# Last stage of an attention, experts and mixing kernel: theta three tiles ahead in the first batch

## The chip, the cores and the metric

The kernel runs on one core of a Trainium2 chip. The metric is the device time in microseconds (us). TensorE (PE in the profile) multiplies matrices and writes to PSUM, a memory of eight banks of 128 x 512 floats; VectorE (DVE), ScalarE (ACT) and GpSimd (POOL) do the elementwise work; SyncE (SP) issues DMAs. Each engine runs its own list of instructions in the order in which it is written and waits on semaphores for the others.

## The reference

Three parts follow one another: attention with a local band, a mixture of experts, and the stage that the change is in. That one is, for x of 2 x 768 x 512:

```python
def _moe2_ref(x, w_theta, w_tok_r, w_tok_i, w_ch):
    theta = x @ w_theta
    cos_t, sin_t = (np.cos(theta), np.sin(theta))
    zr = x * cos_t
    zi = x * sin_t
    yr = np.einsum('ts,bsd->btd', w_tok_r, zr)
    yi = np.einsum('ts,bsd->btd', w_tok_i, zi)
    y = yr + yi
    u = x + y
    return (u + np.maximum(u @ w_ch, 0.0)).astype(np.float32)
```

## The kernel before

The last stage works on `NT` = 12 tiles of 128 tokens, `QT` = 6 for each of the two batches. Products are made exact enough by splitting every operand into a high and a low part (`exact`, line 1192: three matmuls, high x high and the two mixed ones, for each piece). ScalarE writes the high part, VectorE subtracts it from the whole for the low part.

For one tile n the work goes:

- VectorE `weigh(n)` (line 958): multiplies the gathered rows by the expert's probability, in `x_tok`.
- PE `turn_x2(n)` (L1243): four transposes of the tile into PSUM bank 6.
- ACT `x_high(n)` (L634) and DVE `x_low(n)` (L961): the halves `x2T_hi`, `x2T_lo`, two buffers each.
- PE `theta(n)`: 12 matmuls of 512 columns (`wth_hi`, `wth_lo` with `x2T_hi`, `x2T_lo`) into bank 7.
- DVE `reduce_angle(n)` (L988 to L995, "the angles" below): six dependent instructions that read bank 7 and bring theta into a range for the sine. Its last one counts `s_e_rr`.
- ACT `rotation(n)` (L640, L641, L643): Abs and two Sin; DVE `rotate(n)` (L968): x times cosine and sine; inside it stands `weigh(n + 2)`; ACT `z_high(n)` (L648), DVE z_lo (L961).
- PE `mix(n, 0)` and `mix(n, 1)`: 18 matmuls each, the tile's part of the token mix for all six output tiles of its batch, accumulated in banks 0 to 5.

When a batch's six tiles are mixed, VectorE adds x (`add_y`, L1001), PE turns u (`turn_u`, L1281), its halves are made (`u_high`, `u_low`), and `channels(n)` multiplies by w_ch; `finish` (L1006) writes the output tile. The weights of the token mix are split too, one block of 128 rows of both matrices at a time (`weights_high(m)`, L663 and L664, `weights_low(m)`), w_ch last (m = 6).

The order is written out by hand in each engine's list. PE begins with turn_x2(0), theta(0), turn_x2(1), theta(1), turn_x2(2). Then step s is: mix(s, 0); turn_u(s - 6) from s = 6 on; theta(s + 2); turn_x2(s + 3); mix(s, 1); channels(s - 6). VectorE's step s, which starts from -2, works with m = s + 2: reduce_angle(m), x_low(m + 1), weights_low(m + 1) while m is 2 to 5, rotate(m). For m = 0 and 1 the weight split stands behind rotate. ScalarE's list has the same form. `theta(n)` waits for `s_e_rr` at n, that is for the angles of tile n - 1, since all thetas share bank 7.

Of the kernel before, what the change touches and what calls it, by code (L numbers as in the profile page):

```python
# [25 lines left out]
P = 128  # L26
# [96 lines left out]
def channel_bank(n):  # L123

    return 7 if n < QT else n % QT

# [7 lines left out]
def program(nc, q2, kx, vx, n_global, n_local, w_gates, w_experts, w_theta, w_tok_rT, w_tok_iT, w_ch,  # L134
# [5 lines left out]
    with ExitStack() as ctx:  # L140
# [402 lines left out]
        def _(act):  # L543
# [87 lines left out]
            def x_high(n):  # L631
                act.wait_ge(s_e_tx, n + 1)
                wait(act, s_e_th, n - 1)
                act.copy(x2T_hi[:, n % 2, :, :], ps[:, 6, :].rearrange("p (c q) -> p c q", c=DC)).then_inc(s_e_xh, 1)  # L634
# [34 lines left out]

            act.activation(ang_a[:, 0:1], half_pi[:, 0:1], ACT.Sin)  # L670
            x_high(0)
            weights_high(0)
            for s in range(-2, NT):
                m, n = s + 2, s - QT
                if n >= 0:
                    u_high(n)
                if m + 1 < NT:
                    x_high(m + 1)
                if 2 <= m < QT:
                    weights_high(m + 1)  # L680
                if m < NT:
                    rotation(m)
                    z_high(m)
                if m < 2:
                    weights_high(m + 1)
# [5 lines left out]
        def _(dve):  # L691
# [271 lines left out]
            def rotate(n):  # L963

                dve.wait_ge(s_e_trig, 2 * (n + 1))
                wait(dve, s_e_zl, n)
                for m in range(2):
                    dve.tensor_tensor(z[:, m, :], x_tok[:, n, :], trig[:, m, :], ALU.mult).then_inc(s_e_z, 1)  # L968
                if n + 2 < NT:
                    weigh(n + 2)  # L970
                dve.wait_ge(s_e_z, 2 * (n + 1))
                dve.wait_ge(s_e_zh, n + 1)
                low(z_lo[:, n % 2, :, :], z[:], z_hi[:, n % 2, :, :]).then_inc(s_e_zl, 1)

            def x_low(n):
                dve.wait_ge(s_e_xh, n + 1)
                low(x2T_lo[:, n % 2, :, :], ps[:, 6, :].rearrange("p (c q) -> p c q", c=DC), x2T_hi[:, n % 2, :, :]).then_inc(s_e_xl, 1)
# [6 lines left out]
            def reduce_angle(n):  # L984
                dve.wait_ge(s_e_th, n + 1)
                th = ps[:, 7, :]
# [31 lines left out]
            low(wth_lo[:], wth[:], wth_hi[:]).then_inc(s_w_lo, 1)  # L1018
            weigh(0)
            weigh(1)  # L1020
            x_low(0)
            weights_low(0)
            for s in range(-2, NT):
# [5 lines left out]
                if m + 1 < NT:  # L1029
                    x_low(m + 1)  # L1030
# [3 lines left out]
                if 2 <= m < QT:  # L1034
                    weights_low(m + 1)
                if m < NT:
                    rotate(m)
                if m < 2:
                    weights_low(m + 1)
# [13 lines left out]
        def _(pe):  # L1053
# [184 lines left out]
            def turn_x2(n):  # L1238
                pe.wait_ge(s_x2, n + 1)
                wait(pe, s_e_xl, n)  # L1240
                wait(pe, s_e_ul, n - QT - 2)
                for c in range(DC):
                    last = pe.transpose(ps[:, 6, c * P:(c + 1) * P], x_tok[:, n, c * P:(c + 1) * P], ident)  # L1243
                last.then_inc(s_e_tx, 1)

            def theta(n):
                pe.wait_ge(s_e_xl, n + 1)
                wait(pe, s_e_rr, n)
# [3 lines left out]
                exact(ps[:, 7, :], [((x2T_hi[:, n % 2, c, :], x2T_lo[:, n % 2, c, :]), (wth_hi[:, c, :], wth_lo[:, c, :]))  # L1252
                                    for c in range(DC)], True, True).then_inc(s_e_th, 1)

            def mix(n, part):
# [7 lines left out]
                for i in range(QT):  # L1263
                    if part == 0 and n == QT:
# [8 lines left out]
            def turn_u(n):  # L1273
                pe.wait_ge(s_e_u, n + 1)
                if n < QT:
                    pe.wait_ge(s_e_xl, min(n + QT + 3, NT))
# [19 lines left out]
            for n in range(2):  # L1296
                theta(n)
                turn_x2(n + 1)
            for s in range(NT):
# [3 lines left out]
                if s + 2 < NT:  # L1303
                    theta(s + 2)
                if s + 3 < NT:
                    turn_x2(s + 3)
# [55 lines left out]
```

## Time and profile before

| what | us |
|---|---|
| median of 3 runs | 564.17 |
| lowest, highest | 562.51, 564.87 |
| the profiled execution | 563.1 |
| its span in the trace | 561.2 |
| PE busy in the span | 496.5 |
| DVE busy | 287.0 |
| ACT busy | 197.0 |

The profile is of one execution. Busy time is the time in which an engine executes; matmuls are pipelined and overlap their neighbours, so the start of one to the start of the next tells what it costs. "Idle before" in a row is the time in which the engine did nothing, with the work that ended the wait. The granted clock is the share of 2.4 GHz that TensorE had: 1.00 is 2.4 GHz, 0.50 is 1.2 GHz.

The last stage begins when the rows of the experts have come back, about 365 us into the span, and lasts to the end.

### The profile page before, as it was taken

The numbers are of one execution on the slowest core, as the hardware profiler recorded it, in microseconds if no ns is written. First come the engines' busy times: TensorE is split into PE (matmuls) and PEld (weight loads), VectorE is DVE, ScalarE is ACT, GpSimd is POOL, SyncE is SP. The second block draws the span as 40 slices with busy tenths as digits, with TensorE's granted clock in tenths as the row PEclk, the third lists the DMA queues.
The fourth block names the chain that finished last, engine by engine and source line by source line (L and its number), as shares of the span: only waits on it lengthen the run. The fifth ranks groups of instructions, "written<-read, shape, count | busy, mean of one in ns | idle before, by whom it ended". The sixth has DMA issues, their size and how long they took to land.

```text
span 561.2 us, 9141 instructions
## 1 busy us (share of the span) xinstructions
PE 496.5 (88%) x3228; PEld 420.0 (75%) x3229; DVE 287.0 (51%) x641; ACT 197.0 (35%) x411; POOL 113.3 (20%) x111
## 2 busy tenths in 40 slices
PE   0799999922699999999999999558999999999987
PEld 0577777711699999999899899446888878888866
DVE  5577887546411514141442531257988685655053
ACT  2588877602011313131423411334544322222010
POOL 3977773000111222121222211000000000000000
PEclk9999999965699999999999999877999999999999
DMA  7533344476331547382992800150000000000012
GB/s 268 201 137 107 118 145 161 189 255 273 107 110 39 227 182 277 136 339 76 380 378 76 347 36 19 33 196 0 1 0 2 0 0 20 20 19 20 19 39 94
DMA packets 19842, 70.76 MB, mean 126 GB/s; under 512 B 3038, under 2 KB 3294, under 8 KB 15712
## 3 DMA queue, kind: packets, MB, share of 16 engines
q1 hardware_dynamic: 16880, 64.05, 30.0%
q0 software_dynamic: 2640, 6.30, 3.2%
q8 instruction: 17, 0.28, 0.2%
q14 instruction: 17, 0.14, 0.1%
q10 hardware_dynamic: 288, 0.00, 0.0%
HBM read 62.21 MB, written 10.49 MB: 130 GB/s over the span
## 4 chain that ended last, share of the span: by engine, by line
PE 80%; DVE 8%; DMA 6%; issue 3%; ACT 1%; SPq 0%; POOLq 0%; DVEq 0%; POOL 0%
PE ps L1192 42%; PE ps L1220 18%; PE ps L1066 5%; PE ps L1124 5%; PE ps L1108 4%; DMA w_sb<-in_w_experts 4%; PE ps L1088 3%; PE ps L1206 1%; PE ps L1281 1%; PE ps L1243 1%; DMA xin<-x_rows,rows_in 1%; DVE glob L723 1%; DMA x_tok<-y_rows 0%; PE ps L1199 0%; SPq L437 0%
## 5 line engine op out<-in xcount | busy, mean ns | idle before, releaser
L1220 PEld LDWEIGHTS ps<-xT,w_sb 128*128 128x128 f32 x1024 | 118.2, 194 | 3.8 <-issue 1.4
L1220 PE MATMUL ps<-xT,w_sb 128*128 128x128 f32 x1024 | 118.8, 277 | 1.6 <-DVE xT L950 1.0
L936 DVE SCALAR_TENSOR_TENSOR hT_lo<-ps,hT_hi 128x512 fp32r<-128x512 f32 x32 | 22.1, 691 | 101.1 <-ACT hT_hi L613 101.0
L945 DVE TENSOR_TENSOR w_lo<-w_sb,w_hi 128x1024 fp32r<-128x1024 f32 x32 | 37.0, 1220 | 39.0 <-ACT w_hi L624 39.0
L1192 PE MATMUL ps<-w_hi,hT_hi 128*128 128x512 f32 x128 | 51.5, 402 | 0.0
L567 ACT ACTIVATE prob<-raw,row_min 128x256 f32<-128x256 f32 (+1 forms) x96 | 46.2, 484 | 13.4 <-DVE row_min L786 12.3
L1192 PE MATMUL ps<-w_hi,hT_lo 128*128 128x512 f32 x128 | 50.1, 391 | 0.0
L1192 PE MATMUL ps<-w_lo,hT_hi 128*128 128x512 f32 x128 | 49.9, 390 | 0.0
L613 ACT ACTIVATE hT_hi<-ps 128x512 fp32r<-128x512 f32 x32 | 19.1, 598 | 83.1 <-PE ps L1220 83.1
L617 ACT COPY yout<-ps 128x512 f32<-128x512 f32 x16 | 9.4, 587 | 85.2 <-PE ps L1192 85.2
L786 DVE CUSTOM_DVE_ANT_0 raw<-ps,levels 128x256 f32<-128x256 f32 (+1 forms) x96 | 33.8, 394 | 4.8 <-PE ps L1066 4.8
L624 ACT CAST w_hi<-w_sb 128x1024 fp32r<-128x1024 f32 x32 | 31.1, 1046 | 12.8 <-DVE slot_part L906 12.8
L1066 PE MATMUL ps<-k_hi,q_hi 64*128 64x256 f32 (+1 forms) x96 | 19.1, 394 | 16.9 <-POOL k_lo L492 15.8
L492 POOL TENSOR_TENSOR k_lo<-k_raw,k_hi 128x1344 fp32r<-128x1344 f32 (+1 forms) x16 | 28.9, 1829 | 14.1 <-ACT k_hi L552 14.1
L1124 PE MATMUL ps<-probT,v_sb 128*64 128x128 f32 x352 | 30.5, 291 | 0.2
L1108 PE MATMUL ps<-cst,prob 128*128 128x128 f32 x176 | 30.1, 292 | 0.2 <-ACT prob L567 0.2
L1192 PE MATMUL ps<-z_hi,wti_hi 128*128 128x512 f32 x72 | 29.2, 405 | 0.0
L1192 PE MATMUL ps<-z_hi,wtr_hi 128*128 128x512 f32 x72 | 28.2, 392 | 0.6 <-DVE x_tok L1001 0.6
L1066 PEld LDWEIGHTS ps<-k_hi,q_hi 64*128 64x128 f32 x96 | 9.6, 196 | 24.9 <-issue 20.5
L1192 PE MATMUL ps<-z_hi,wti_lo 128*128 128x512 f32 x72 | 28.2, 392 | 0.0
L1192 PE MATMUL ps<-z_lo,wti_hi 128*128 128x512 f32 x72 | 28.1, 390 | 0.0
L1192 PE MATMUL ps<-z_hi,wtr_lo 128*128 128x512 f32 x72 | 28.0, 389 | 0.0
(185 smaller groups left out, 948.6 us busy)
## 6 DMA issues: line engine op xcount, KB each, us to landing
w_sb<-in_w_experts SPq DMA_DIRECT2D x32, 1024.0 KB
v_sb<-in_vx SPq DMA_DIRECT2D x8, 640.0 KB, 4.0
k_raw<-in_kx SPq DMA_DIRECT2D x8, 432.0 KB, 5.4
q_raw<-in_q SPq DMA_DIRECT2D x8, 384.0 KB, 6.0
x_rows<-x_tok SPq DMA_DIRECT2D x2, 1536.0 KB, 8.9
x_tok<-y_rows SPq DMA_DIRECT2D x12, 256.0 KB, 5.2
out_x<-o_sb SPq DMA_DIRECT2D x12, 256.0 KB, 2.0
wtr<-in_w_tok_rT SPq DMA_DIRECT2D x6, 384.0 KB
```

The source lines that it names most:

```text
L492: last_part = pool.tensor_tensor(low, whole, high.bitcast(F32), ALU.subtract)
L567: act.activation(where, of, ACT.Exp, bias=row_min[:, m:m + 1], scale=-1.0, accum_out=den[:, h % 2, i, b:b + 1]).then_inc(s_exped, 1)
L613: act.activation(hT_hi[:, 4 * half:4 * half + 4, :], ps[:, 1 + half, :].rearrange("p (c q) -> p c q", c=4), ACT.Relu).then_inc(high, 1)
L624: act.copy(w2_hi_quarter(q), quarter(w_sb, par, q)).then_inc(s_w2_hi, 1)
L786: dve.tensor_tensor_reduce(raw[:, g % 2, b * WINDOW:b * WINDOW + w], ps[:, 2 * (g % 2) + b, 0:w], levels[:, h, min(i, 1), 0:w], -DH ** -0. ...
L936: dve.scalar_tensor_tensor(hT_lo[:, part, :], ps[:, 1 + half, :].rearrange("p (c q) -> p c q", c=4), 0.0, hT_hi[:, part, :].bitcast(F32), ...
L945: dve.tensor_tensor(quarter(w_lo, par, q), quarter(w_sb, par, q), w2_hi_quarter(q).bitcast(F32), ALU.subtract).then_inc(s_w2_lo, 1)
L1066: last = pe.matmul(bank, of[d, r, i * P:(i + 1) * P], part, start=(m == 0), stop=(m == 2))
L1108: last = pe.transpose(ps[:, 4 + r, c], prob[:, r, c], ident)
L1124: last = pe.matmul(ps[b * DH:(b + 1) * DH, 6, (i % GROUP) * P:(i % GROUP + 1) * P], v_sb[:, h % 2, b, block, :], probT[:, r, b * WINDOW + ...
L1192: last = pe.matmul(bank, a, b, start=(start and j == 0 and m == 0), stop=(stop and j == count - 1 and m == 2))
L1220: last = pe.matmul(ps[:, 1 + half, f * P:(f + 1) * P], w_sb[:, par, c // 2, j:j + P], xT[:, c, :], start=(c == 0), stop=(c == DC - 1))
```

## The change

The change alters the lists of PE, ACT and DVE in the last stage. Everything ahead of it is the same.

- PE's list begins with turn_x2(0), turn_x2(1), theta(0), turn_x2(2), theta(1), theta(2), turn_x2(3). In steps 0 to 5 it has theta(s + 3) and turn_x2(s + 4), in step 6 neither, and from step 7 on the same as before.
- theta(1) writes bank 5 and turn_x2(1) bank 4. These are banks of the mix, so the first mix waits before bank 5 until the angles of tile 1 are reduced. All other thetas stay in bank 7, all other turns in bank 6.
- theta(1) does not wait for `s_e_rr`, theta(2) waits for 1, and theta(n) from 3 on for n, as before.
- DVE's list: the split of the first weight block comes ahead of the first `weigh`; three tiles are weighed at the start, and `rotate(n)` weighs tile n + 3; x_low of the tile that `x2_at(s)` names (m + 2 in the first batch) comes behind reduce_angle(m), then the weight split, then the rotation. ACT's list follows.

```diff
--- before.py
+++ after.py
@@ -123,6 +123,26 @@
 def channel_bank(n):
 
     return 7 if n < QT else n % QT
+
+
+def theta_bank(n):
+
+    return 5 if n == 1 else 7
+
+
+def x2_bank(n):
+
+    return 4 if n == 1 else 6
+
+
+def theta_at(s):
+
+    return [s + 3] if s < QT else [s + 2] if QT < s < NT - 2 else []
+
+
+def x2_at(s):
+
+    return [s + 4] if s < QT else [s + 3] if QT < s < NT - 3 else []
 
 
 def wait(eng, sem, value):
@@ -631,7 +651,7 @@
             def x_high(n):
                 act.wait_ge(s_e_tx, n + 1)
                 wait(act, s_e_th, n - 1)
-                act.copy(x2T_hi[:, n % 2, :, :], ps[:, 6, :].rearrange("p (c q) -> p c q", c=DC)).then_inc(s_e_xh, 1)
+                act.copy(x2T_hi[:, n % 2, :, :], ps[:, x2_bank(n), :].rearrange("p (c q) -> p c q", c=DC)).then_inc(s_e_xh, 1)
 
             def rotation(n):
 
@@ -667,22 +687,24 @@
                     act.copy(wch_hi[:], wch[:]).then_inc(s_w_hi, 1)
 
 
+            weights_high(0)
             act.activation(ang_a[:, 0:1], half_pi[:, 0:1], ACT.Sin)
             x_high(0)
-            weights_high(0)
+            x_high(1)
+            weights_high(1)
+            x_high(2)
             for s in range(-2, NT):
                 m, n = s + 2, s - QT
                 if n >= 0:
                     u_high(n)
-                if m + 1 < NT:
-                    x_high(m + 1)
-                if 2 <= m < QT:
+                if m:
+                    for ahead in x2_at(s):
+                        x_high(ahead)
+                if 0 < m < QT:
                     weights_high(m + 1)
                 if m < NT:
                     rotation(m)
                     z_high(m)
-                if m < 2:
-                    weights_high(m + 1)
             for n in range(QT, NT):
                 u_high(n)
 
@@ -966,15 +988,15 @@
                 wait(dve, s_e_zl, n)
                 for m in range(2):
                     dve.tensor_tensor(z[:, m, :], x_tok[:, n, :], trig[:, m, :], ALU.mult).then_inc(s_e_z, 1)
-                if n + 2 < NT:
-                    weigh(n + 2)
+                if n + 3 < NT:
+                    weigh(n + 3)
                 dve.wait_ge(s_e_z, 2 * (n + 1))
                 dve.wait_ge(s_e_zh, n + 1)
                 low(z_lo[:, n % 2, :, :], z[:], z_hi[:, n % 2, :, :]).then_inc(s_e_zl, 1)
 
             def x_low(n):
                 dve.wait_ge(s_e_xh, n + 1)
-                low(x2T_lo[:, n % 2, :, :], ps[:, 6, :].rearrange("p (c q) -> p c q", c=DC), x2T_hi[:, n % 2, :, :]).then_inc(s_e_xl, 1)
+                low(x2T_lo[:, n % 2, :, :], ps[:, x2_bank(n), :].rearrange("p (c q) -> p c q", c=DC), x2T_hi[:, n % 2, :, :]).then_inc(s_e_xl, 1)
 
             def u_low(n):
                 dve.wait_ge(s_e_uh, n + 1)
@@ -983,7 +1005,7 @@
 
             def reduce_angle(n):
                 dve.wait_ge(s_e_th, n + 1)
-                th = ps[:, 7, :]
+                th = ps[:, theta_bank(n), :]
                 wait(dve, s_e_trig, 2 * (n - 1))
                 then(dve.tensor_scalar(ang_k[:], th, float(1 / (2 * np.pi)), MAGIC, ALU.mult, ALU.add))
                 then(dve.tensor_scalar(ang_k[:], ang_k[:], MAGIC, None, ALU.subtract))
@@ -1016,27 +1038,28 @@
 
             dve.wait_ge(s_w_hi, 1)
             low(wth_lo[:], wth[:], wth_hi[:]).then_inc(s_w_lo, 1)
+            weights_low(0)
             weigh(0)
             weigh(1)
+            weigh(2)
             x_low(0)
-            weights_low(0)
+            x_low(1)
+            weights_low(1)
             for s in range(-2, NT):
                 m, n = s + 2, s - QT
                 if n >= 0:
                     u_low(n)
                 if m < NT:
                     reduce_angle(m)
-                if m + 1 < NT:
-                    x_low(m + 1)
+                for ahead in x2_at(s):
+                    x_low(ahead)
                 if s == QT - 1:
                     for i in range(QT):
                         add_y(i)
-                if 2 <= m < QT:
+                if 0 < m < QT:
                     weights_low(m + 1)
                 if m < NT:
                     rotate(m)
-                if m < 2:
-                    weights_low(m + 1)
                 if n >= 0:
                     finish(n)
             add_y(QT)
@@ -1237,19 +1260,21 @@
 
             def turn_x2(n):
                 pe.wait_ge(s_x2, n + 1)
-                wait(pe, s_e_xl, n)
-                wait(pe, s_e_ul, n - QT - 2)
+                if n > 1:
+                    pe.wait_ge(s_e_xl, n if n > 2 else 1)
+                wait(pe, s_e_ul, n - QT - 2 if n > QT + 3 else 0)
                 for c in range(DC):
-                    last = pe.transpose(ps[:, 6, c * P:(c + 1) * P], x_tok[:, n, c * P:(c + 1) * P], ident)
+                    last = pe.transpose(ps[:, x2_bank(n), c * P:(c + 1) * P], x_tok[:, n, c * P:(c + 1) * P], ident)
                 last.then_inc(s_e_tx, 1)
 
             def theta(n):
                 pe.wait_ge(s_e_xl, n + 1)
-                wait(pe, s_e_rr, n)
+                if n > 1:
+                    pe.wait_ge(s_e_rr, n if n > 2 else 1)
                 wait(pe, s_e_o, n - QT - 2)
                 if n == 0:
                     pe.wait_ge(s_w_lo, 1)
-                exact(ps[:, 7, :], [((x2T_hi[:, n % 2, c, :], x2T_lo[:, n % 2, c, :]), (wth_hi[:, c, :], wth_lo[:, c, :]))
+                exact(ps[:, theta_bank(n), :], [((x2T_hi[:, n % 2, c, :], x2T_lo[:, n % 2, c, :]), (wth_hi[:, c, :], wth_lo[:, c, :]))
                                     for c in range(DC)], True, True).then_inc(s_e_th, 1)
 
             def mix(n, part):
@@ -1261,6 +1286,8 @@
                     if b == 0:
                         pe.wait_ge(s_w_lo, n + 2)
                 for i in range(QT):
+                    if part == 0 and n == 0 and i == theta_bank(1):
+                        pe.wait_ge(s_e_rr, 2)
                     if part == 0 and n == QT:
                         pe.wait_ge(s_e_u, i + 1)
                     q = slice(i * P, (i + 1) * P)
@@ -1273,7 +1300,7 @@
             def turn_u(n):
                 pe.wait_ge(s_e_u, n + 1)
                 if n < QT:
-                    pe.wait_ge(s_e_xl, min(n + QT + 3, NT))
+                    pe.wait_ge(s_e_xl, min(max(n, 1) + QT + 3, NT))
                 wait(pe, s_e_ul, n if n <= QT else n - 1)
                 if n > QT:
                     pe.wait_ge(s_e_o, QT)
@@ -1293,17 +1320,20 @@
                        for c in range(DC)], True, True).then_inc(s_e_v, 1)
 
             turn_x2(0)
-            for n in range(2):
-                theta(n)
-                turn_x2(n + 1)
+            turn_x2(1)
+            theta(0)
+            turn_x2(2)
+            theta(1)
+            theta(2)
+            turn_x2(3)
             for s in range(NT):
                 mix(s, 0)
                 if s >= QT:
                     turn_u(s - QT)
-                if s + 2 < NT:
-                    theta(s + 2)
-                if s + 3 < NT:
-                    turn_x2(s + 3)
+                for ahead in theta_at(s):
+                    theta(ahead)
+                for ahead in x2_at(s):
+                    turn_x2(ahead)
                 mix(s, 1)
                 if s >= QT:
                     channels(s - QT)
```

The order of TensorE's instructions at the start of the stage, before (`x_tok` is turned, `wth` times `x2T` is theta):

```order
L1243 MATMUL ps<-cst,x_tok 128x128 [waits x2]
L1243 MATMUL ps<-cst,x_tok 128x128 x3
L1192 MATMUL ps<-wth_hi,x2T_hi 128x512 [waits w_lo,e_xl]
L1192 MATMUL ps<-wth_lo,x2T_hi 128x512
L1192 MATMUL ps<-wth_hi,x2T_lo 128x512
```

and in the changed kernel:

```order
L1267 MATMUL ps<-cst,x_tok 128x128 [waits x2]
L1267 MATMUL ps<-cst,x_tok 128x128 x3
L1267 MATMUL ps<-cst,x_tok 128x128 [waits x2]
L1267 MATMUL ps<-cst,x_tok 128x128 x3
L1215 MATMUL ps<-wth_hi,x2T_hi 128x512 [waits w_lo,e_xl]
```

A second turn has come between the first and theta(0).

TensorE at the end of mix(0, 0), before, where theta(2) follows:

```order
L1192 MATMUL ps<-z_hi,wtr_hi 128x512
L1192 MATMUL ps<-z_lo,wtr_hi 128x512
L1192 MATMUL ps<-z_hi,wtr_lo 128x512
L1192 MATMUL ps<-wth_hi,x2T_hi 128x512 [waits e_rr,e_xl]
L1192 MATMUL ps<-wth_lo,x2T_hi 128x512
```

and in the changed kernel, where theta(3) follows:

```order
L1215 MATMUL ps<-z_lo,wtr_hi 128x512
L1215 MATMUL ps<-z_hi,wtr_lo 128x512
L1215 MATMUL ps<-z_hi,wtr_hi 128x512 [waits e_rr]
L1215 MATMUL ps<-z_lo,wtr_hi 128x512
L1215 MATMUL ps<-z_hi,wtr_lo 128x512
L1215 MATMUL ps<-wth_hi,x2T_hi 128x512 [waits e_rr,e_xl]
L1215 MATMUL ps<-wth_lo,x2T_hi 128x512
```

The rows at the end are alike; what moved is the tile. The wait `e_rr` of the last rows is for 2 before and for 3 in the change, and the mix has a wait of its own ahead of its last three matmuls.

VectorE from x_low of the first step (s = -2) on, before (`z` is the rotation's product, `ang` the angles):

```order
L961 TENSOR_TENSOR x2T_lo<-ps,x2T_hi 128x512 [waits e_xh]
L968 TENSOR_TENSOR z<-x_tok,trig 128x512 [waits e_trig]
L968 TENSOR_TENSOR z<-x_tok,trig 128x512
L958 TENSOR_SCALAR x_tok<-x_tok,p_sel 128x512 [waits gathered2]
L961 TENSOR_TENSOR z_lo<-z,z_hi 128x1024 [waits e_zh,e_z]
L961 TENSOR_TENSOR wtr_lo<-wtr,wtr_hi 128x768 [waits w_hi]
L961 TENSOR_TENSOR wti_lo<-wti,wti_hi 128x768
L988 TENSOR_SCALAR ang_k<-ps 128x512 [waits e_th]
```

and in the changed kernel:

```order
L983 TENSOR_TENSOR x2T_lo<-ps,x2T_hi 128x512 [waits e_xh]
L990 TENSOR_TENSOR z<-x_tok,trig 128x512 [waits e_trig]
L990 TENSOR_TENSOR z<-x_tok,trig 128x512
L980 TENSOR_SCALAR x_tok<-x_tok,p_sel 128x512 [waits gathered3]
L983 TENSOR_TENSOR z_lo<-z,z_hi 128x1024 [waits e_zh,e_z]
L1010 TENSOR_SCALAR ang_k<-ps 128x512 [waits e_th]
L1011 TENSOR_SCALAR ang_k<-ang_k 128x512 [waits ch]
L1013 SCALAR_TENSOR_TENSOR ang<-ang_k,ps 128x512 [waits ch]
L1015 SCALAR_TENSOR_TENSOR ang<-ang_k,ang 128x512 [waits ch]
L1016 SCALAR_TENSOR_TENSOR ang<-ang_k,ang 128x512 [waits ch]
L1017 TENSOR_SCALAR ang<-ang 128x512 [waits ch]
L983 TENSOR_TENSOR x2T_lo<-ps,x2T_hi 128x512 [waits e_xh]
```

The weight split (`wtr_lo`, `wti_lo`) of this place has moved ahead; the angles follow z_lo directly. The first `x2T_lo` is of tile 1 before and of tile 2 in the change, and the last row is the one of tile 3.

## Rows read from the trace of the kernel before

**Rows 1.** The page's first line: span and instructions
```profile
span 561.2 us, 9141 instructions
```
**Rows 2.** Waits of TensorE, 366 to 562 us: total, times, longest
```profile
PE ps L1192 <- DVE x2T_lo L961: 7.4, 3, 4.0
```
**Rows 3.** Timeline of PE: start us, us, line, operation, shape, count, [idle before]
```profile
377.16 0.50 PE L1192 MATMUL ps<-wth_hi,x2T_hi 128*128 128x512 f32 x1 [4.04 <-DVE x2T_lo L961]
...
382.10 0.50 PE L1192 MATMUL ps<-z_hi,wtr_hi 128*128 128x512 f32 x1
...
388.39 0.72 PE L1192 MATMUL ps<-wth_hi,x2T_hi 128*128 128x512 f32 x1 [1.95 <-DVE x2T_lo L961]
...
393.20 0.48 PE L1192 MATMUL ps<-z_hi,wti_hi 128*128 128x512 f32 x1
...
401.48 0.39 PE L1192 MATMUL ps<-wth_hi,x2T_hi 128*128 128x512 f32 x1
...
404.20 0.60 PE L1243 MATMUL ps<-cst,x_tok 128*128 128x128 f32 x4
...
450.05 0.48 PE L1192 MATMUL ps<-z_hi,wti_hi 128*128 128x512 f32 x1
...
466.96 0.39 PE L1192 MATMUL ps<-wch_hi,uT_hi 128*128 128x512 f32 x1
```
**Rows 4.** Busy time by stretch of the last stage, PEclk the granted clock
```profile
365.60:368.10 2.50, 1.11 (x4) 0.71 (x4) 1.18 (x2) 1.34 (x3) 0.00 (x0) 0.50 0.98 320
373.10:377.10 4.00, 0.02 (x1) 0.00 (x0) 3.83 (x7) 1.15 (x3) 0.00 (x0) 1.00 0.00 0
377.10:378.30 1.20, 1.14 (x5) 0.97 (x6) 0.00 (x1) 1.20 (x3) 0.00 (x0) 0.98 0.07 14
378.30:381.50 3.20, 3.20 (x9) 2.36 (x8) 2.38 (x4) 1.84 (x3) 0.00 (x0) 0.50 0.00 0
386.40:388.40 2.00, 0.05 (x2) 0.01 (x1) 1.87 (x4) 0.62 (x2) 0.00 (x0) 1.00 0.00 0
388.40:391.50 3.10, 3.10 (x8) 2.42 (x9) 1.69 (x3) 1.74 (x4) 0.00 (x0) 0.52 0.00 0
```
**Rows 5.** Timeline of ACT, same columns as rows 3
```profile
376.54 0.63 ACT L640 ACTIVATE ang_a<-ang 128x512 f32<-128x512 f32 x1 [2.80 <-DVE ang L995]
...
404.83 0.59 ACT L634 CAST x2T_hi<-ps 128x512 fp32r<-128x512 f32 x1 [1.25 <-PE ps L1243]
...
405.32 0.84 ACT L663 CAST wtr_hi<-wtr 128x768 fp32r<-128x768 f32 x1
...
406.06 0.83 ACT L664 CAST wti_hi<-wti 128x768 fp32r<-128x768 f32 x1
...
408.65 0.64 ACT L640 ACTIVATE ang_a<-ang 128x512 f32<-128x512 f32 x1 [1.76 <-DVE ang L995]
...
428.06 1.92 ACT L667 CAST wch_hi<-wch 128x2048 fp32r<-128x2048 f32 x1
```
**Rows 6.** Timeline of DVE, same columns as rows 3
```profile
378.33 1.29 DVE L968 TENSOR_TENSOR z<-x_tok,trig 128x512 f32<-128x512 f32 x2 [1.23 <-ACT trig L643]
...
380.81 1.23 DVE L961 TENSOR_TENSOR z_lo<-z,z_hi 128x1024 fp32r<-128x1024 f32 x1 [0.79 <-ACT z_hi L648]
...
403.69 1.22 DVE L961 TENSOR_TENSOR z_lo<-z,z_hi 128x1024 fp32r<-128x1024 f32 x1 [0.79 <-ACT z_hi L648]
...
404.83 0.68 DVE L988 TENSOR_SCALAR ang_k<-ps 128x512 f32<-128x512 f32 x1
...
409.13 0.95 DVE L961 TENSOR_TENSOR wtr_lo<-wtr,wtr_hi 128x768 fp32r<-128x768 f32 x1
...
410.00 0.95 DVE L961 TENSOR_TENSOR wti_lo<-wti,wti_hi 128x768 fp32r<-128x768 f32 x1
...
431.45 2.28 DVE L961 TENSOR_TENSOR wch_lo<-wch,wch_hi 128x2048 fp32r<-128x2048 f32 x1
...
454.20 3.67 DVE L1001 TENSOR_TENSOR x_tok<-ps,x_tok 128x512 f32<-128x512 f32 x6
```

## The prediction

> **What bounds the kernel now.** I read the page's head first, then the waits of TensorE in the last stage, then the last stage in order of time on TensorE, VectorE and ScalarE, and at last the granted clock of single stretches. One execution spans 561.2 us and its time is 563.1 us, 1.9 outside the span [rows 1]. From 366 us on TensorE lacks work in few places: 7.4 us in three waits for a low half of the turned x (`x2T_lo`) [rows 2]. Two of the three lie where the change works: theta(1) starts at 377.16 after 4.04 idle, theta(2) at 388.39 after 1.95 [rows 3]. From mix(0,1) at 393.20 to mix(5,1) at 450.05, five steps, TensorE is dense: 56.85 / 5 = 11.37 us a step [rows 3]. The clock reads 1.00 in the idle 2.0 us before 388.4 and 0.52 in the 3.1 us behind it; after the 4.0 us idle it is 0.98 for 1.2 us and 0.50 for 3.2; after the 7.4 us idle at the start it is 0.50 as well [rows 4]. So behind each idle stretch about 3.2 us of matmuls ran at 1.2 GHz instead of 2.4, about 1.6 to 1.7 us lost each time.
>
> **The opening.** What is hoisted costs nothing: the first weight split goes before the first gathered tile, where TensorE waits for `x_tok` anyhow. turn_x2(1) goes beside ScalarE's and VectorE's work between turn_x2(0) and theta(0), a gap in which TensorE idles. Theta(1) no longer waits for the first angles, since its bank is 5; theta(2), behind it in bank 7, does: it takes the slot at 377.16 that theta(1) had. That removes one theta from later, and the long idle before it. But mix(0,0) waits for z_lo(0), which hangs on theta(0), angles(0) and the rotation, and none of these moves; z_lo starts at 380.81 [rows 6], mix(0,0) at 382.10 [rows 3] in both kernels. So the gain of the opening isn't banked at mix(0,0); it would be at theta(2)'s old place.
>
> **The loop the change closes.** Bank 7 holds every theta from 2 on. Theta(3), behind mix(0,0) in TensorE's order, must wait for the angles of tile 2 (`s_e_rr` at 3). Before, theta(2) stood there and wanted the angles of tile 1 alone. In general, step s now runs theta(s+3), which wants angles(s+2), and behind it turn_x2(s+4). On VectorE x_low(s+4) stands ahead of the weight split, of rotate(s+2) and so of angles(s+3), for which theta(s+4) waits. Every link waits for the one before, so one step of TensorE can't be shorter than the sum:
> - theta start to x_high start 3.35 (401.48 to 404.83) [rows 3, 5];
> - x_high and two casts of ScalarE 0.49 + 2 x 0.74 = 1.97, then Abs to the rotation's product 1.79 (376.54 to 378.33) [rows 5, 6]: 7.1. VectorE's own leg: the casts end at about 5.4, then two splits 0.87 apart [rows 6], 7.2. The later counts: 7.2;
> - product to z_lo 2.48 (378.33 to 380.81), z_lo to the next angles 1.14 (403.69 to 404.83), angles to their end 3.82 (404.83 to 408.65) [rows 5, 6].
>
> That is 14.6 us against TensorE's 11.37. In the step with w_ch the cast takes 1.92 and the split 2.2 [rows 5, 6], so the product comes at 3.35 + 0.49 + 1.92 + 2.2 = 8.0 and the loop is 15.4; in the step without weights the product comes at 5.6 and the loop is 13.1. Before, theta(s+3) needed angles(s+2) as well, but these ran while TensorE did mixes, and x_low stood only behind a turn that had been issued before; nothing in a step waited for the next theta but its own angles.
>
> **The sum.** Angles(1) start 381.95 (380.81 + 1.14), end 385.77. x_low(3) 0.6 and two splits 1.74 put the product at 388.0; + 2.48 + 1.14 + 3.8 makes angles(2) end and theta(3) start at 395.4. (Mix(0,0) itself waits some 0.3 in its last bank for angles(1), inside the same gap.) TensorE, done with mix(0,0) at about 386.7, idles 8.7 us. From there five loops: 3 x 14.64 + 15.4 + 13.1 = 72.4, so theta(8) starts at 467.8 and mix(5,1) 3.07 later (theta 2.72, turn 0.35) at 470.9, 20.8 us later than before. Given back: theta(8) and turn_x2(9), once in step 6, are done. Before, channels(0) came 16.9 us after mix(5,1) began (450.05 to 466.96) [rows 3]. Before, VectorE was still at angles(7) when the banks were ready and made the six additions in one piece, 3.67 us from 454.20 on [rows 6]. Now it is idle there: the additions follow the banks (the last matmul at 4.15, one addition 0.6 to 0.7) and end at 5.0; product to z_lo and its own time, 2.48 + 1.14, make 8.6; turn_u(0) at 8.3 and its halves (0.6, 0.6, 0.6) 10.1; angles(8) end at 13.9, and channels(0) waits for these: 3.0 back. Behind this both kernels have the same order and TensorE is dense. Net at full clock: +17.8.
>
> The clock on top. Theta(3) follows 8.7 us idle and would run at 1.2 GHz: its 12 matmuls and the turn 2.8 more (as theta(0) after 7.4 idle, whose clock was 0.50) [rows 4]. Theta(4) to theta(7) follow idles of 14.6 - 11.4 = 3.2 and once 4.0; the row after 1.95 and the one after 4.04 both lost 1.7 in the next theta, 4 x 1.7 = 6.8, and since theta is a link of the loop, that lengthens the loop. Theta(8) follows 1.7, I count nothing (else 1.7). Not shown by the trace is a stall of that size in every step; bounds from the nearest rows: 0 below (dense stretches show 1.00) and 1.7 on six thetas above. I take 9.6. The sum is +27.4: 563.1 + 27.4 = 590.5, and since the median of the runs shown is 1.1 above the profiled one, 591.
>
> The Trainium skill (TensorE: Matmul & The Clock Gate, HAM oscillation) has the same thing at work where a matmul stream is interrupted at every repetition: the clock falls back each time. The row after 1.95 us idle agrees [rows 4]; the sum above holds without the page.
>
> **The rivals.**
> 1. The stall is paid once. VectorE needs less than TensorE for a tile (in the steady part it waits for theta), so after theta(3) it might stay ahead. Then mix(0,1) starts at 398.5 or with the slow clock 401.3 instead of 393.20: 5 to 8, less what step 6 returns: about 570. Against it: x_low(s+4) can't start before turn_x2(s+4), and rotation and angles are queued behind it. 5%.
> 2. The loop as computed, but the clock stays at 2.4 GHz behind stalls of 3.2 us: 17.8 + 2.8 = 20.6, so 585; against it is the row after 1.95 idle. 18%.
> 3. The clock spreads into the mixes so that TensorE's own work, not only theta, passes the loop: 14.6 + 1.7 against 8.7 us of other work at half clock, 17.4 + 5.5: up to 6 more in some steps; 600 and over. 6%.
> 4. Faster: the look-ahead holds. If theta(3) needed no bank that VectorE still has to read, it would follow mix(0,0) at 386.7 and mix(0,1) start at 389.8 instead of 393.20: 3.4 less, so 561. It decides on the row of theta(3): idle below 2 us. For it: nothing but that x_low(3) is done by then. The Trainium skill (Perfetto Trace Analysis, Optimizing Tensor Performance) advises to rotate independent matmul groups through different PSUM banks so that the reading of one lies beside the next; by it the own bank of theta(1) is a gain. No trace here shows two thetas side by side, and from theta(2) on one bank is used. 4%.
>
> The forecast has 67%.
>
> **How the numbers follow.** 591 is the forecast's; its own spread is the clock's (0 to 1.7 for each of the last thetas, 588 to 594). The range takes in rival 2 and a part of rival 3: 582 to 597. What a measurement of this kernel can tell from no change is about 0.5%, 2.8 us. Slower holds the forecast and rivals 1 to 3 and is 0.95; faster is rival 4, 0.04; same 0.01.
>
> **What would show it.** Right: after mix(0,0) TensorE idles 8 to 9 us for the angles (`ang`), then about 3 us in each of the next four or five steps, always ahead of a theta; the sum of TensorE's waits for the angles is near 25 us; theta starts 16 to 17 us apart; VectorE waits for `x2T_hi` in each step; behind channels(0) nothing differs. Wrong: idle ahead of theta(3) alone (rival 1), a clock of 1.00 in thetas behind stalls (rival 2), slow mixes (rival 3), no wait for the angles (rival 4), or a start of mix(0,0) other than near 382.

## The result, and the profile after

| | before | after |
|---|---|---|
| median of 4 runs, us | 563.98 | 592.28 |
| lowest to highest | 562.51 to 564.87 | 591.49 to 594.42 |
| span of the profiled execution | 561.2 | 592.6 |

The ratio is 1.051, 95% interval 1.048 to 1.054. The forecast was 591.

The first views of the changed kernel to read are the page's first line and TensorE's waits in the last stage (waiting line, then who it waited for: total, times, longest):

```profile
span 592.6 us, 9139 instructions
```
```profile
PE ps L1215 <- DVE ang L1017: 24.6, 6, 8.8
...
PE ps L1215 <- DVE x2T_lo L983: 2.3, 2, 1.3
```

Before, this view had 7.4 us in waits for low halves of the turned x [rows 2] and no entry for the angles. Now it waits six times, 24.6 us in all, for the angles (L1017 is their last instruction). The timeline of TensorE shows where:

```profile
369.07 1.97 PE L1267 MATMUL ps<-cst,x_tok 128*128 128x128 f32 x8 [7.29 <-DVE x_tok L980]
...
385.86 0.50 PE L1215 MATMUL ps<-z_hi,wtr_hi 128*128 128x512 f32 x1 [1.37 <-DVE z_lo L983]
...
399.28 0.77 PE L1215 MATMUL ps<-wth_hi,x2T_hi 128*128 128x512 f32 x1 [8.76 <-DVE ang L1017]
...
415.53 0.47 PE L1215 MATMUL ps<-wth_hi,x2T_hi 128*128 128x512 f32 x1 [3.20 <-DVE ang L1017]
...
431.95 0.47 PE L1215 MATMUL ps<-wth_hi,x2T_hi 128*128 128x512 f32 x1 [3.21 <-DVE ang L1017]
...
448.37 0.47 PE L1215 MATMUL ps<-wth_hi,x2T_hi 128*128 128x512 f32 x1 [3.22 <-DVE ang L1017]
...
464.00 0.76 PE L1215 MATMUL ps<-wth_hi,x2T_hi 128*128 128x512 f32 x1 [4.00 <-DVE ang L1017]
...
479.35 0.47 PE L1215 MATMUL ps<-wth_hi,x2T_hi 128*128 128x512 f32 x1 [2.23 <-DVE ang L1017]
...
498.16 0.47 PE L1215 MATMUL ps<-wch_hi,uT_hi 128*128 128x512 f32 x1 [1.01 <-issue]
```

Each wait for L1017 stands ahead of a theta, the first after 8.76 us, then 3.20, 3.21, 3.22, 4.00 and 2.23. These rows answer to those of [rows 3]: mix(0,0) at 385.86 (382.10 before), channels(0) at 498.16 (466.96).

The span of the profiled execution grew by 31.4 us, the median by 28.3. In parts:

| part of the span | before | after | difference |
|---|---|---|---|
| start to the first turn | 365.61 | 369.07 | 3.46 |
| first turn to mix(0,0) | 16.49 | 16.79 | 0.30 |
| mix(0,0) to channels(0) | 84.86 | 112.30 | 27.44 |
| channels(0) to the end | 94.24 | 94.44 | 0.20 |

The 3.46 isn't the change's. Only the hoisted weight split stands ahead of the first turn, and behind it VectorE still waits 0.27 us for the DMA that brings the first tile. The start of the first turn varies from one execution to the next: it came between 364.5 and 370.0 in the ten profiled executions here that open in this way or nearly so. (The profiled execution of the changed kernel is its longest, 594.42.) What the change did is the third line.

One step of the loop on VectorE and ScalarE, from the timelines of the changed kernel:

```profile
404.15 0.59 ACT L654 CAST x2T_hi<-ps 128x512 fp32r<-128x512 f32 x1 [10.04 <-PE ps L1267]
...
406.11 0.63 ACT L660 ACTIVATE ang_a<-ang 128x512 f32<-128x512 f32 x1
...
409.30 1.05 ACT L668 CAST z_hi<-z 128x1024 fp32r<-128x1024 f32 x1 [1.43 <-DVE z L990]
```
```profile
398.71 0.43 DVE L1017 TENSOR_SCALAR ang<-ang 128x512 f32<-128x512 f32 x1
...
404.77 0.69 DVE L983 TENSOR_TENSOR x2T_lo<-ps,x2T_hi 128x512 fp32r<-128x512 f32 x1 [5.64 <-ACT x2T_hi L654]
...
407.99 1.28 DVE L990 TENSOR_TENSOR z<-x_tok,trig 128x512 f32<-128x512 f32 x2
...
410.46 1.23 DVE L983 TENSOR_TENSOR z_lo<-z,z_hi 128x1024 fp32r<-128x1024 f32 x1 [0.79 <-ACT z_hi L668]
...
411.60 0.68 DVE L1010 TENSOR_SCALAR ang_k<-ps 128x512 f32<-128x512 f32 x1
...
414.95 0.43 DVE L1017 TENSOR_SCALAR ang<-ang 128x512 f32<-128x512 f32 x1
```

VectorE ends the angles at 399.14 and then waits 5.64 us for the high half of a tile whose turn TensorE issues only behind the theta that these very angles let go. Then split (beside it the casts on ScalarE, ahead of Abs at 406.11), product, z_lo and the next angles follow with hardly a gap, and theta(4) starts at 415.53, 0.14 behind their end.

The granted clock (PEclk, the third column from the right; the first pair of columns is PE's busy time):

```profile
399.30:402.90 3.60, 3.60 (x10) 2.88 (x11) 0.00 (x0) 0.00 (x0) 0.00 (x0) 0.58 0.00 0
403.60:415.50 11.90, 8.73 (x41) 6.93 (x40) 8.87 (x13) 4.77 (x7) 0.00 (x0) 1.00 0.00 0
415.50:419.90 4.40, 4.37 (x12) 3.45 (x13) 0.00 (x0) 0.00 (x0) 0.00 (x0) 0.61 0.01 4
448.40:451.20 2.80, 2.80 (x13) 2.27 (x14) 0.00 (x0) 0.00 (x0) 0.00 (x0) 1.00 0.00 0
```

Thetas behind a stall mostly ran partly at 1.2 GHz (0.58 and 0.61), the mixes behind them at 2.4. Theta(6), at 448.37, ran at 2.4 throughout although 3.22 us of idle stood ahead of it, as ahead of theta(5).

### The profile page after: what moved, and what is told of

Read it like the earlier page. It is cut to its first block, busy times and chain, and to the rows that moved or that the text cites. A ratio compares the mean times of both kernels' runs of the same rounds, so it can differ in the third digit from the quotient of the medians.

```text
span 592.6 us, 9139 instructions
## 1 busy us (share of the span) xinstructions
PE 506.5 (85%) x3228; PEld 425.6 (72%) x3229; DVE 287.3 (48%) x641; ACT 196.7 (33%) x411; POOL 113.3 (19%) x111
## 4 chain that ended last, share of the span: by engine, by line
PE 72%; DVE 12%; DMA 6%; issue 6%; ACT 3%; SPq 1%; DVEq 0%; POOLq 0%; POOL 0%; ACTq 0%
PE ps L1215 35%; PE ps L1243 17%; PE ps L1089 5%; PE ps L1147 4%; PE ps L1131 4%; DMA w_sb<-in_w_experts 4%; PE ps L1111 3%; DVE z L990 1%; ACT z_hi L668 1%; PE ps L1229 1%; DVE ang L1016 1%; DVE ang L1015 1%; DVE ang L1013 1%; DVE ang_k L1010 1%; PE ps L1308 1%
## 5 line engine op out<-in xcount | busy, mean ns | idle before, releaser
L1215 PE MATMUL ps<-wth_hi,x2T_hi 128*128 128x512 f32 x48 | 23.4, 488 | 26.9 <-DVE ang L1017 24.6
L1215 PEld LDWEIGHTS ps<-wth_hi,x2T_hi 128*128 128x128 f32 x48 | 11.0, 230 | 32.3 <-issue 27.0
L1089 PE MATMUL ps<-k_hi,q_hi 64*128 64x256 f32 (+1 forms) x96 | 19.5, 402 | 16.8 <-POOL k_lo L512 15.8
L1131 PE MATMUL ps<-cst,prob 128*128 128x128 f32 x176 | 31.5, 302 | 0.2 <-ACT prob L587 0.2
L654 ACT CAST x2T_hi<-ps 128x512 fp32r<-128x512 f32 x12 | 7.0, 587 | 71.9 <-PE ps L1267 71.8
```

The costliest lines, as they stand in the source:

```text
L1089: last = pe.matmul(bank, of[d, r, i * P:(i + 1) * P], part, start=(m == 0), stop=(m == 2))
L1131: last = pe.transpose(ps[:, 4 + r, c], prob[:, r, c], ident)
L1215: last = pe.matmul(bank, a, b, start=(start and j == 0 and m == 0), stop=(stop and j == count - 1 and m == 2))
```

## The experiments

Nine kernels, one of them run twice. Each result is a median with its lowest and highest, then its ratio to the kernel before, run beside it, with the 95% interval. The kernel before had medians of 564.2 to 565.6 there. Idle times, starts and step lengths are from one profiled execution of each kernel. Where a diff is said to be abridged, it shows only the calls that move.

### The loop's second branch: x_low behind the rotation

Abridged (the weight split stays where it was, ahead of the rotation):

```diff
 # ACT, steps 0 to 4
-                    for ahead in x2_at(s): x_high(ahead)
                     rotation(m)
                     z_high(m)
+                    for ahead in x2_at(s): x_high(ahead)
 # DVE, steps 0 to 4
-                for ahead in x2_at(s): x_low(ahead)
                 weights_low(m + 1)
                 rotate(m)
+                for ahead in x2_at(s): x_low(ahead)
```

> The changed kernel (592.3), but in steps 0 to 4 VectorE's x_low(s+4) and ScalarE's x_high(s+4) stand behind the rotation and its split instead of ahead of it. Theory A (the loop has two branches; with x_low out of the way it goes on through the buffers of z: z_high(s+2) waits for the end of mix(s,1), and behind it come z_lo, x_low, angles(s+3), theta(s+4)): theta start 2.72 + 0.35 to mix(s,1), 4.15 for it, 1.05 + 0.1 + 1.14 for z, 0.6 for x_low, 3.8 for the angles = 14.0 a step instead of 14.6, TensorE still idle about 2.8 ahead of each theta: 2 to 4 us faster than the change, 588 to 590. Theory B (x_low ahead of the rotation is all that closes the loop): the stall is paid once, at theta(3), and steps are 11.4 long: about 20 us faster, 570 to 573.

Measured: 589.04 (586.29 to 591.52), 1.044 of before (1.040 to 1.048). Theory A. TensorE in this kernel (the waits for the angles ahead of theta(4), theta(5) and theta(6); those ahead of theta(7) and theta(8) are 2.83 too, that ahead of theta(3) 8.77):

```profile
410.27 0.47 PE L1223 MATMUL ps<-wth_hi,x2T_hi 128*128 128x512 f32 x1 [2.83 <-DVE ang L1021]
...
426.31 0.47 PE L1223 MATMUL ps<-wth_hi,x2T_hi 128*128 128x512 f32 x1 [2.83 <-DVE ang L1021]
...
440.77 0.47 PE L1223 MATMUL ps<-wth_hi,x2T_hi 128*128 128x512 f32 x1 [2.83 <-DVE ang L1021]
```
```profile
433.95 1.05 ACT L668 CAST z_hi<-z 128x1024 fp32r<-128x1024 f32 x1 [5.99 <-PE ps L1223]
```

Every step still has an idle, 2.83 instead of 3.2, and ScalarE waits 5.99 us for the mix before z_high. A step was 14.46 where theta ran at 2.4 GHz (426.31 to 440.77) and 16.0 where it didn't (410.27 to 426.31). The sum had 14.0; z_high came 7.64 behind theta's start (426.31 to 433.95), where the sum had 7.2. So x_low ahead of the rotation isn't the only way in which the loop closes: behind it, z_high(s+2) waits for mix(s,1), since z has two buffers.

### Both branches open

Abridged:

```diff
 # ACT, steps -1 to 5: weights_high, rotation(m),
+                    for ahead in x2_at(s): x_high(ahead)
                     z_high(m)
 # DVE, steps -1 to 5: weights_low, product of tile m, weigh,
+                    for ahead in x2_at(s): x_low(ahead)
+                    reduce_angle(m + 1)
                     z_lo of tile m
```

The angles' old place, at the start of a step, falls away but for tile 1; in step 5 the additions of x stand in place of the angles.

> The changed kernel, still three ahead with bank 7 for every theta from 2 on, but with other orders in steps -1 to 5: ScalarE splits weights, rotates tile m, makes x_high(s+4), and only then z_high(m); VectorE splits weights, makes the product of tile m, weighs, makes x_low(s+4), reduces the angles of tile m+1, and only then makes z_lo(m). Both branches of the loop are open then: the angles of the next tile wait neither for the rotation behind x_low nor for z_high and mix(s,1). Theory A (the order of VectorE's and ScalarE's work around one bank closes the loop, not the look-ahead as such): one stall ahead of theta(3), 5 to 8 us, steps of 11.4 behind it: 567 to 571, 21 to 25 faster than the change, yet slower than two ahead (557.8). Theory B (three ahead through one bank can't be fed in any order): 585 or more.

Measured: 568.02 (566.17 to 572.8), 1.008 of before (1.004 to 1.012). Theory A: its only wait for the angles is

```profile
394.29 0.77 PE L1235 MATMUL ps<-wth_hi,x2T_hi 128*128 128x512 f32 x1 [6.94 <-DVE ang L1025]
```

and behind it theta(4) to theta(8) start 11.4 apart (407.3, 418.7, 430.1, 441.5, 452.8). The same look-ahead through the same bank costs 24 us less once the angles of the next tile stand neither behind x_low and the rotation nor behind z_high. z_high itself still waits for the mix in each of these steps (3.6 us of ScalarE's idle), which now holds up nothing that theta needs. What is left against the kernel before, in the profiled executions: 1.25 us from the first turn to mix(0,0), where theta(0) took 5.29 us, all at 1.2 GHz, against 4.39, and 2.4 us from mix(0,0) to channels(0), where TensorE idles 6.94 us ahead of theta(3) against 1.95 ahead of theta(2) before.

### The split behind the rotation

Abridged:

```diff
-                if 0 < m < QT: weights_low(m + 1)   # and weights_high on ACT
                 rotate(m)
+                if 0 < m < QT: weights_low(m + 1)
```

> The changed kernel with the split of the token weights (and w_ch) behind the rotation on both engines instead of ahead of it. Theory A (what counts is the whole chain from theta to the next angles; behind the rotation the split is still ahead of the next angles, and its cast now waits for z_high, so the chain is up to 1 us longer in four steps, with more clock loss at the idle): 3 to 8 us slower than the change, 595 to 600. Rival (the split ahead of the rotation is what makes the loop too long): some 1.5 us less in each of four steps, 586.

Measured: 599.95 (598.01 to 603.83), 1.065 of before (1.058 to 1.071): theory A. The idle ahead of theta(4) is 4.24 instead of 3.20:

```profile
416.65 0.47 PE L1215 MATMUL ps<-wth_hi,x2T_hi 128*128 128x512 f32 x1 [4.24 <-DVE ang L1017]
```

Within the changed kernel the place of the split that it chose is the better one; it is not what costs.

### A longer link, in both kernels

```diff
+                for _ in range(2):
+                    then(dve.tensor_scalar(a, a, PI_BELOW, -PI_BELOW, ALU.min, ALU.max))
                 dve.tensor_scalar(a, a, PI_BELOW, -PI_BELOW, ALU.min, ALU.max).then_inc(s_e_rr, 1)
```

> The changed kernel with two more clamps, 0.46 us each, at the end of the angles of every tile (the same clamp repeated). Theory A (the angles lie on the loop in every step): +0.92 for each of nine tiles up to angles(8), 8.3, and where channels(n) wait for the angles in the second batch, 1 to 2 more: 10 us slower, 602 (to 605 with the clock's share). Rival (VectorE's work hides under TensorE except once): +0.9 to 3, 593 to 595.

> The kernel before with the same two extra clamps (0.92 us a tile) in the angles. Theory A (in the kernel before the angles are on the path only for tiles 0 and 1, and a little in the second batch where channels(n) wait for them): 2 x 0.92 and 1 to 2 more, with the clock's share 3 to 6 us, 567 to 570, against the 17 that they cost in the changed kernel. Rival (VectorE's angles bound both kernels alike): 12 or more.

Measured: 609.44 (606.79 to 613.14) with the change, 17.2 above its 592.28; as ratios to before 1.077 (1.071 to 1.083) against 1.051, which makes 14.6. The kernel before with the clamps: 569.34 (566.76 to 573.71), 1.010 of before (1.006 to 1.013), 5.2 above the 564.18 beside it. The rivals fall, but the changed kernel lost more than the 10 to 13 expected. Idle ahead of theta(4) and theta(5), and ahead of channels(0):

```profile
423.15 0.47 PE L1217 MATMUL ps<-wth_hi,x2T_hi 128*128 128x512 f32 x1 [4.16 <-DVE ang L1019]
...
440.50 0.47 PE L1217 MATMUL ps<-wth_hi,x2T_hi 128*128 128x512 f32 x1 [4.12 <-DVE ang L1019]
...
511.76 0.47 PE L1217 MATMUL ps<-wch_hi,uT_hi 128*128 128x512 f32 x1 [1.93 <-issue]
```

A step is 17.35 (423.15 to 440.50), 0.93 more than 16.42 (415.53 to 431.95): the loop's part is as computed. Where the rest lies, from the timelines of the profiled executions, each against its kernel without the clamps:

| what the clamps' kernel has more, us | changed kernel | kernel before |
|---|---|---|
| start to the first turn | 0.9 | 0.3 |
| first turn to mix(0,0) | 2.7 | 0.8 |
| mix(0,0) to channels(0) | 10.0 | 2.3 |
| channels(0) to the end | 5.1 | 3.7 |
| together | 18.7 | 7.1 |

The third line is where the two kernels' orders differ most, and it decides between theory and rival: 10.0 against 2.3. It has the eight angles' worth that the sum had there (7.4) and 2.6 of clock: theta(3) and theta(7) took 5.3 us, all 12 matmuls at 1.2 GHz (4.2 and 4.3 without the clamps), theta(6) 4.4 (2.8), and against that theta(8) 2.8 (4.0). The first two lines hold things that the clamps can't have done: theta(0), which no angles stand ahead of, took 5.3 us (4.2), and the DMA of the third tile landed later. In the last line 1 to 2 was expected in both kernels. Both have 1.6 of clock in channels(6), 4.4 us instead of 2.9, and the changed kernel 1.5 more in channels(0), which now waits 1.93 and took 4.4 (2.8). So of the 17 us the loop's share is the computed 7.4; the rest is clock, the second batch and what varies between executions.

### TensorE kept at work in its stalls

```diff
 def theta(n):
                 pe.wait_ge(s_e_xl, n + 1)
+                if 3 <= n <= 8:
+                    for j in range(34 if n == 3 else 12):
+                        pe.matmul(ps[:, 6, :], x2T_hi[:, n % 2, j % DC, :], wth_hi[:, j % DC, :],
+                                  start=True, stop=True)
                 if n > 1:
                     pe.wait_ge(s_e_rr, n if n > 2 else 1)
```

> The changed kernel, but TensorE does spare matmuls into bank 6 (34 of 512 columns ahead of theta(3), 12 ahead of each of theta(4) to theta(8)) behind the wait for x_low and ahead of the wait for the angles, so that it works through its stalls; their results are overwritten. Theory A (a part of the loss, some 8 us, is theta at 1.2 GHz behind each stall; the thetas 3 to 8 of the changed kernel took 4.2, 4.4, 4.3, 2.8, 4.3 and 4.0 us instead of 2.7): all of them 2.7 to 2.8, a step 14.6 instead of 16.3, time 7 to 8 us less, 584 to 586. Rival (the clock costs nothing, the loop alone sets the step, or the spare work is late and costs what it saves): 592 or more.

Measured: 586.46 (585.54 to 587.17), 1.038 of before (1.035 to 1.042); 5.8 less than the change by the medians, 7 by the ratios. Its thetas (two stretches) and a step between them:

```profile
396.40:399.20 2.80, 2.76 (x12) 2.30 (x13) 0.00 (x0) 0.00 (x0) 0.00 (x0) 1.00 0.00 0
399.30:411.10 11.80, 11.53 (x53) 9.26 (x51) 8.81 (x13) 4.77 (x7) 0.00 (x0) 1.00 0.01 1
411.20:414.00 2.80, 2.78 (x12) 2.31 (x13) 0.00 (x0) 0.00 (x0) 0.00 (x0) 1.00 0.00 0
```
```profile
411.22 0.50 PE L1215 MATMUL ps<-wth_hi,x2T_hi 128*128 128x512 f32 x1 [0.39 <-DVE ang L1017]
...
425.99 0.50 PE L1215 MATMUL ps<-wth_hi,x2T_hi 128*128 128x512 f32 x1 [0.39 <-DVE ang L1017]
```

All at 1.00, and a step is 14.77, 0.13 above the 14.64 of the sum. The spare matmuls end before the angles do (TensorE still idles 0.39), so they don't cause the 0.13; theta took 2.86 here against 2.72 in the row that the sum used. Only ahead of theta(8) are they late, by 0.4. From mix(0,0) to channels(0) this kernel took 104.60 us, 7.7 less than the change (112.30) and 19.7 more than the kernel before (84.86). The first is the clock's share, about what was expected; the second is the loop and its first stall, at full clock.

### Two ahead behind the new opening

```diff
 def theta_at(s):
-    return [s + 3] if s < QT else [s + 2] if QT < s < NT - 2 else []
+    return [s + 2] if 0 < s < NT - 2 else []
 def x2_at(s):
-    return [s + 4] if s < QT else [s + 3] if QT < s < NT - 3 else []
+    return [s + 4] if s < 0 else [s + 3] if 0 < s < NT - 3 else []
```

and the two waits that belong to it (turn_x2(n) for `s_e_ul`, turn_u(n) for `s_e_xl`) as in the kernel before.

> The changed kernel with its opening, own banks and hoisted work, but from then on theta two ahead: step 0 has no theta and no turn, step 1 has theta(3) and turn_x2(4), and so on as in the kernel before. Theory A (the third tile of look-ahead in the loop is what costs, the opening is a gain): mix(0,0) starts as before, theta(3) waits for nothing but the angles of tile 2, which end while TensorE runs mix(0,1) and mix(1,0); mix(1,1) starts about 399 against 404.55 before, 5 to 6 us sooner, and the lead stays to the end: 558 to 559, 33 faster than the change. Rival (the opening and the own banks cost too, or the lead is lost at the batch boundary): 564 or more.

Measured: 557.81 (557.75 to 561.09), 0.989 of before (0.985 to 0.994): faster than both kernels. TensorE in this kernel:

```profile
365.41 1.97 PE L1267 MATMUL ps<-cst,x_tok 128*128 128x128 f32 x8 [7.41 <-DVE x_tok L980]
...
382.20 0.50 PE L1215 MATMUL ps<-z_hi,wtr_hi 128*128 128x512 f32 x1 [1.37 <-DVE z_lo L983]
...
391.85 0.50 PE L1215 MATMUL ps<-z_hi,wtr_hi 128*128 128x512 f32 x1 [0.89 <-DVE z_lo L983]
...
396.07 0.39 PE L1215 MATMUL ps<-wth_hi,x2T_hi 128*128 128x512 f32 x1
...
399.15 0.48 PE L1215 MATMUL ps<-z_hi,wti_hi 128*128 128x512 f32 x1
```

Mix(1,1) starts at 399.15, 33.7 behind the first turn; before it was 38.9 (365.61 to 404.55). The angles of tile 2 are made while TensorE does mix(0,1) and mix(1,0), and theta(3) at 396.07 waits for nothing.

Run again, beside the last kernel below:

> The two-ahead kernel with the new opening once more, beside the one above: 557.8, which is 1.1% below the kernel before.

561.76 (556.51 to 564.50), 0.994 of before (0.991 to 0.997). The sign holds; the gain is 0.6% instead of 1.1%, and the intervals overlap. Of the 3.4 us between the profiled executions of the two runs, 0.8 lie ahead of the first turn, 1.1 are theta(0), all at 1.2 GHz (5.3 us; 4.2 in the first), and 1.4 are channels(6) in the second batch (4.3 us; 2.9 in the first). How often each comes in unprofiled runs isn't known.

### The opening's parts

Theta(1) in bank 7:

```diff
 def theta_bank(n):
-    return 5 if n == 1 else 7
+    return 7
```

with the waits that go with it (every theta(n) for `s_e_rr` at n, none inside mix(0,0)).

> The kernel with the new opening and theta two ahead from step 1 on (557.8), but theta(1) in bank 7 like the others, so it waits for the angles of tile 0 and theta(2), which stands ahead of mix(0,0), for those of tile 1. Theory A (the own bank is what makes the opening a gain): mix(0,0) starts 6 to 7 us later, 564 to 565, level with the kernel before. Rival (the hoisted work and the early turn are the gain, the bank is worth little): 558 to 560.

Measured: 567.63 (565.22 to 571.23), 1.006 of before (1.003 to 1.010). Theory A in its direction, but 3 above its number. From the timeline of the profiled execution mix(0,0) starts 26.0 behind the first turn against 16.8; the expectation left out that theta(2), behind 5.0 us of idle, runs at 1.2 GHz too. The own bank of theta(1) is worth at least the opening's whole gain.

Tile 2 weighed behind x_low(0):

```diff
-            weigh(2)
             x_low(0)
+            weigh(2)
             x_low(1)
```

> The two-ahead kernel with the new opening (557.8), but VectorE weighs tile 2 behind x_low(0) instead of ahead of it: in the changed kernel's opening x_low(0) stood behind a tile whose DMA landed late (x_low(0) at 371.32 where its high half was done at 370.81), and theta(0) started 2.99 us behind the first turn instead of 2.52. Theory: theta(0) starts 0.3 to 0.5 us sooner and mix(0,0) with it, 557.3 to 557.8, too little to tell from run to run; the trace shows the distance from the first turn to mix(0,0), 16.8 us, shrink to 16.3 to 16.5. Rival: the gathered tile is late for the third turn as well and nothing moves.

Measured: 558.67 (558.38 to 561.26), 0.990 of before (0.987 to 0.993). In time it can't be told from the kernel without it. In the trace x_low(0) starts 1.77 behind the first turn, where it was 2.27:

```profile
369.86 0.69 DVE L983 TENSOR_TENSOR x2T_lo<-ps,x2T_hi 128x512 fp32r<-128x512 f32 x1 [1.17 <-ACT x2T_hi L654]
...
370.47 0.48 DVE L980 TENSOR_SCALAR x_tok<-x_tok,p_sel 128x512 f32<-128x512 f32 x1
```
```profile
367.28 0.49 DVE L980 TENSOR_SCALAR x_tok<-x_tok,p_sel 128x512 f32<-128x512 f32 x1 [1.31 <-DMA x_tok<-y_rows]
...
367.68 1.28 DVE L983 TENSOR_TENSOR x2T_lo<-ps,x2T_hi 128x512 fp32r<-128x512 f32 x2
```

In the second fence, the order of the change, VectorE sits 1.31 us at the third tile's DMA with x_low(0) queued behind it. From the first turn to mix(0,0) it is 16.5 against 16.8. One execution of each wouldn't show this, but the other kernels with the order of the change do: the longer that wait, the later theta(0). With 0.34 us (below, from the kernel with x_low behind the rotation) theta(0) starts 2.51 behind the first turn, as it does before the change (2.52); with 1.06 us 2.83, with 1.53 us 3.24, with 1.89 us 3.65.

```profile
365.42 0.49 DVE L984 TENSOR_SCALAR x_tok<-x_tok,p_sel 128x512 f32<-128x512 f32 x1 [0.34 <-DMA x_tok<-y_rows]
```

## Why the prediction was right

By its own steps:

- **The opening.** Mix(0,0) was said to stay where it is. It came 0.30 later against the first turn. The sum had hoisting at nothing. Theta(0) started 0.47 later, since weigh(2) stands ahead of x_low(0) and waited 1.27 for its DMA, and itself took 0.18 less (4.21 against 4.39). In an execution in which that DMA landed early, theta(0) wasn't late (last experiment), so the term at nothing holds in some executions and not in others.
- **The stall ahead of theta(3).** Worked out 8.7 us, and theta(3) 13.3 behind mix(0,0); measured 8.76 and 13.42.
- **The loop.** 14.6 at full clock, 16.3 with the clock's 1.7; measured 16.25, 16.42 and 16.42 for the three steps with split token weights, whose thetas were slow, and 14.77 where TensorE was kept at work. The step with w_ch was 15.4 in the sum and 15.63 measured, its theta at full clock. For the last step the sum had 13.1; it was 15.35, of which theta(7)'s clock is 1.6 and 0.6 a link that the sum missed: ScalarE's z_high(6) waited for the end of mix(4,1). The chain of waits of the changed kernel has it:

```profile
468.90 4.15 PE ps L1215 x18
...
473.13 1.06 ACT z_hi L668
...
474.28 0.06 DVE z_lo L983
```

- **What is given back.** 3.0 in step 6, with channels(0) 13.9 behind mix(5,1). Measured 14.09 (484.07 to 498.16), so 2.8. Its idle of 1.01 has no releaser in the row, but the angles of tile 8 end at 498.06, 0.10 ahead of it.
- **The clock.** 9.6 in the sum; the thetas 3 to 8 took 4.24, 4.42, 4.34, 2.82, 4.31 and 4.01 against 2.72, together 7.8. Theta(8), counted at nothing, lost 1.3; theta(6), counted at 1.7, 0.1; theta(3) 1.5 of 2.8. The 2.8 came of a misread row: [rows 4] has 0.50 for the stretch of the first turn, not for theta(0), whose own rows are

```profile
368.13 0.79 PE L1192 MATMUL ps<-wth_hi,x2T_hi 128*128 128x512 f32 x1 [1.40 <-DVE x2T_lo L961]
...
372.52 0.60 PE L1243 MATMUL ps<-cst,x_tok 128*128 128x128 f32 x4
```

  that is 4.39 us, 1.7 lost, as behind the shorter idles. Errors of both signs, and keeping TensorE at work returned 5.8 to 7. That the clock falls back at every repetition held for five stalls of six. The section of the Trainium skill that the prediction names for it (TensorE: Matmul & The Clock Gate, HAM oscillation) describes waits of about 3 to 5 us; that 1.95 and 3.2 us can be enough, the rows here show.
- **Mix(0,0) to channels(0)** together: +27.4 in the sum, +27.44 measured. So close is luck in part. Against the sum theta(3) came 0.1 later, the five loops were 1.9 shorter (80.07 against 82.0), theta(8) with its turn 1.65 longer (4.72 against 3.07) and the last part 0.2 longer. At full clock the sum had +17.8, and the kernel with spare matmuls shows +19.7: the sum was 1.9 short in its links and took 1.8 too much for the clock.
- **The last addition.** 563.1 + 27.4 + 1.1 is 591.6; the prediction wrote 591.

Of the rivals, the once-paid stall (1) is the one that could be built: it is the kernel with both branches open, 568.0 where about 570 was said, and it needs another order on two engines. The full clock (2), 585 in the prediction with theta(3) still slow, has no kernel of its own; with theta(3) fast as well, which the sum would put at 582, the kernel with spare matmuls took 586.5. Slow mixes (3) weren't seen: the stretch of mixes from 403.60 to 415.50 reads 1.00. Nor was faster (4).

## What to carry to other kernels

Before letting a producer run one tile further ahead, walk once round the cycle: buffer free, producer, everything that stands behind it in the consumers' queues, buffer free again. If that sum, with the in-order neighbours in it, is longer than the bottleneck engine's step, the look-ahead is paid in every step, not once; a step can have several such cycles (here through the bank of theta and through z's two buffers), and all have to be opened. A look-ahead that only the opening needs can be had in the opening alone.

## What the runs showed of the hardware that I had not expected

The clock of a theta doesn't follow from the idle ahead of it alone: behind 3.21 us theta(5) ran partly at 1.2 GHz (4.34 us), behind 3.22 us theta(6) at 2.4 (2.82), and theta(3) behind 8.76 us lost less (4.24) than in the kernel with the clamps behind 9.69 (5.3). Theta(0), in the same opening, with 7.2 to 7.4 us of idle ahead of the first turns, took 4.2 to 5.3 us from one execution to another.

The fall can come after the engine has started again. The first five matmuls of theta(5) start 0.23 to 0.31 us apart, from the sixth on it is 0.35 and then 0.43:

```profile
432.72 0.39 PE L1215 MATMUL ps<-wth_hi,x2T_hi 128*128 128x512 f32 x1
432.95 0.56 PE L1215 MATMUL ps<-wth_lo,x2T_hi 128*128 128x512 f32 x1
433.30 0.63 PE L1215 MATMUL ps<-wth_hi,x2T_lo 128*128 128x512 f32 x1
```

So which thetas of a kernel would be slow wasn't predictable from the rows of the kernel before; the sum over six of them was, to 2 us, in this one kernel.
